# Four input loads moved to the head of the DMA queue, and two state updates moved ahead of a row split, at the start of the dense layer of a delta-rule and mixture-of-experts kernel

## The reference, cut to what matters

```
y[:, :, t] = einsum('bhd,bhde->bhe', q[:, :, t], state)
v_old = einsum('bhde,bhd->bhe', state, kt)
state = state + bt * einsum('bhd,bhe->bhde', kt, vt - v_old)
```

## Time and profile before

| | |
|---|---|
| median of 3 runs | 976.65 us (973.17, 976.65, 976.8) |
| the profiled execution | 976.8 us, span in the profile 975.1 us |
| PE busy | 922.7 us, 95% of the span |
| DVE, ACT, POOL busy | 459.7, 422.8, 193.9 us |
| DMA | 167.66 MB, mean 172 GB/s |

### The profile page before, as it was taken

The page is one execution under the profiler, slowest core; times in us unless marked ns, Lnnn a source line. Parts: engine busy times, 40 slices in busy tenths (PEclk is TensorE's granted clock), DMA queues, the critical chain, the costliest instruction groups (busy, mean ns, idle before and its releaser), DMA issues.

```text
span 975.1 us, 27207 instructions
## 1 busy us (share of the span) xinstructions
PE 922.7 (95%) x10970; PEld 787.3 (81%) x10971; DVE 459.7 (47%) x948; ACT 422.8 (43%) x765; POOL 193.9 (20%) x146
## 2 busy tenths in 40 slices
PE   4688999999999999999999999976999999999998
PEld 4687778888888788878888888764889899889997
DVE  6999579545855486457522252340232323222221
ACT  4126754654465346544643565511333333333332
POOL 3000000000000000000000052437266633376311
PEclk7689999999999999999999999977899999999999
DMA  7009748543753366435542868137356733362100
GB/s 318 4 27 355 280 164 292 236 131 132 249 214 131 123 223 235 143 120 186 184 153 99 277 226 299 48 138 229 135 205 232 266 129 137 129 260 74 64 22 8
DMA packets 33153, 167.66 MB, mean 172 GB/s; under 512 B 4862, under 2 KB 8100, under 8 KB 27170
## 3 DMA queue, kind: packets, MB, share of 16 engines
q1 hardware_dynamic: 26402, 136.47, 38.9%
q0 software_dynamic: 6560, 29.70, 8.4%
q10 hardware_dynamic: 96, 0.10, 0.0%
HBM read 143.04 MB, written 23.40 MB: 171 GB/s over the span
## 4 chain that ended last, share of the span: by engine, by line
PE 85%; DVE 7%; issue 3%; DMA 2%; ACT 1%; POOL 1%; ACTq 0%; DVEq 0%; POOLq 0%
PE HP L1232 7%; PE ACC L1245 7%; PE HP L1234 6%; PE HP L1233 6%; PE ACC L1246 6%; PE ACC L1247 6%; PE ACC L1651 5%; PE ACC L1650 5%; PE HP L1619 4%; PE ACC L1652 4%; PE HP L1620 4%; PE HP L1621 4%; PE P L1630 3%; PE P L1111 2%; PE P L1138 2%
## 5 line engine op out<-in xcount | busy, mean ns | idle before, releaser
L380 POOL TENSOR_TENSOR we_l<-raw_e,we_h 128x768 fp32r<-128x768 f32 x16 | 29.7, 1870 | 588.7 <-ACT we_h L516 588.7
L482 ACT ACTIVATE relu<-HP 128x512 f32<-128x512 f32 x96 | 57.4, 598 | 203.3 <-PE HP L1234 203.3
L798 DVE TENSOR_TENSOR h_l<-h,h_h 128x512 fp32r<-128x512 f32 x96 | 66.4, 692 | 158.3 <-ACT h_h L490 158.3
L1232 PE MATMUL HP<-x_h,ring 128*128 128x512 f32 x288 | 118.4, 411 | 1.6 <-DVE x_l L791 1.6
L1245 PE MATMUL ACC<-h_h,ring 128*128 128x512 f32 x288 | 116.9, 406 | 2.8 <-DVE h_l L798 2.8
L1233 PE MATMUL HP<-x_h,ring 128*128 128x512 f32 x288 | 113.2, 393 | 0.0
L1234 PE MATMUL HP<-x_l,ring 128*128 128x512 f32 x288 | 113.2, 393 | 0.0
L1246 PE MATMUL ACC<-h_h,ring 128*128 128x512 f32 x288 | 112.5, 391 | 0.0
L1247 PE MATMUL ACC<-h_l,ring 128*128 128x512 f32 x288 | 112.5, 391 | 0.0
L1650 PE MATMUL ACC<-we_h,hT_h 128*128 x240 | 84.7, 353 | 3.6 <-issue 3.4
L1461 POOL TENSOR_TENSOR we_l<-raw_e,we_h 128x1536 fp32r<-128x1536 f32 (+2 forms) x24 | 84.0, 3526 | 19.0 <-DMA we_h<-in_w 18.7
(11 more groups left out here) (222 smaller groups left out, 1723.7 us busy)
## 6 DMA issues: line engine op xcount, KB each, us to landing
ring<-w_scratch SPq DMA_DIRECT2D x80, 768.0 KB, 4.4
raw_e<-in_w SPq DMA_DIRECT2D x16, 1536.0 KB
w_scratch<-ring SPq DMA_DIRECT2D x16, 768.0 KB, 4.4
we_h<-in_w POOLq DMA_DIRECT2D x6, 1536.0 KB, 9.2
kT<-in_kT SPq DMA_DIRECT2D x6, 1024.0 KB, 8.1
kk<-in_k SPq DMA_DIRECT2D x6, 1024.0 KB, 6.7
qT<-in_qT SPq DMA_DIRECT2D x6, 1024.0 KB, 8.3
we_h<-in_w POOLq DMA_DIRECT2D x6, 1024.0 KB, 6.0
```

The costliest lines, as they stand in the source:

```text
L1232: pe.matmul(HP[n % 2][:, :], win_h[:, cols], x_h[:, k, :], start=k == 0, stop=False)
```

## The change

Two lists are reordered; no instruction is added, removed or changed in size.

On SP, the four input loads go ahead of all stores and loads of the weights. The first store and the first load of the loop are taken out of the small loop ahead of it, with the second pair now issued at `i = 0`.

On DVE, the two halves of `new_state(1, g)` are written ahead of `rows_lo(0)` instead of behind it.

```
@@ sync @@
         move_last_heads(sp, (0,))
-        for f in range(2):
-            store_pair(f)
-            load_pair(NPAIR + f)
+        keys_T(2)
+        values(1)
+        queries(1)
+        keys(2)
+        store_pair(0)
+        load_pair(NPAIR)
         for i in range(NF1 * NCH):
             dt, f = divmod(i, NF1)
             t = dt + 1
-            if 0 < i and i + 1 < NF1:
+            if i + 1 < NF1:
                 store_pair(i + 1)
                 if i + 1 + NPAIR < NF1:
                     load_pair(i + 1 + NPAIR)
-            if i == 0:
-                values(1)
-            elif i == 1:
-                keys(2)
-            elif i == 2:
-                keys_T(2)
-            elif i == 3:
-                queries(1)
@@ vector @@
         substitute(1, 9, 20)
-        rows_lo(0)
         for g in range(2):
             new_state(1, g)
+        rows_lo(0)
```

## The result

| | before | changed |
|---|---|---|
| median of 20 runs | 974.48 us (971.82 to 978.19) | 978.48 us (976.27 to 984.99) |
| ratio of the runs | | 1.0058, 95% interval 1.0045 to 1.0073 |
| the profiled execution | 976.8 us, span 975.1 | 982.32 us, span 980.6 |

The prediction was 977.5 and no measurable change, with 0.07 for slower. The median lies inside the range, but the ratio is clear of 1, and its middle is above the 1.005 that I had called the limit of what can be told (the interval reaches down to 1.0045). So the forecast was wrong in kind: the loss is about 5.6 us by the ratio, not 0.85. The same kernel run again in a later comparison gave 1.0038 (1.0022 to 1.0054), 3.7 us: smaller, but again clear of 1.

A forecast was written before the change was run, and what follows sets the result against it. PE, busy 95% of the span, was taken as the bound. Terms -0.1 (hidden inside the 0.65), +0.65 and +0.2 gave +0.85 us: 977.65 on the profiled 976.8, 977.5 against the median 976.65; range 973.0 to 980.1.

The forecast's parts named there:

- What bounds, and what there is to gain: Whole kernel: PE bounds, busy 95%; no engine waits for the four moved loads, so issuing them earlier gives nothing directly.
- (a) DVE's order: Around 73 us, state halves ahead of `rows_lo`: `up(0)` later, `h_l` 0.13 earlier; worth -0.1 us, bounds -0.33 and +0.3.
- the 0.65: Delay in us of `x_l` and `up(0)` from DVE's new order, claimed hidden by PE's following wait for `h_l`.
- (b) The landing of block 4: SP's queue: weight block 4, behind inputs and first store, lands at 86.0 us, bounds 84.5 and 88.5.
- the time until the engines are full: SP's queue: DMA engines full from 72.0 us, 0.9 us after the first issue at 71.14.
- the pace from there on: SP's queue once full: 0.365 MB/us, last engine's lag included, as at the kernel's start; 5.11 MB take until 86.0.
- the prediction's own rule: Block 4's landing delays ACT, then `h_l(2)` and `down(2)` beyond its slack: +0.65 us at 86.0, 3.1 at 88.5.
- What hangs on the landing: `relu(2)` 2.17 us late, `down(2)` +0.65, `below_blocks(1)` +0.2 more; the shift stays to the end.
- The clock: PE's granted clock: no fall in the forecast, longest idle 1.8 us; a fall costing 3.3 us only past about 88.
- the queue starves ACT, and PE's clock falls: Rival: queue at 0.295 MB/us, blocks 4 to 7 late, +4.5 us plus 3.3 from the clock, +7.8, 984.4; chance 0.07.
- The limit of what can be told: Whole kernel time: about 0.5%, 4.9 us, separates a measurable change from none; chance of the same 0.90.

The follow-up runs named there:

- Weights first: Changed kernel with the first store and the load of weight block 4 issued ahead of the four inputs; ratio 1.0011 to the kernel before.
- The dose kernels: Changed kernel with the load of `kk` behind block 4's load: 1.0006; changed kernel with block 1's store and block 5's load ahead of it: 1.0085.
- SP's order alone: Kernel before with only SP's reordering of loads and stores, DVE's list left in its old order; ratio 1.0054.

## Why the prediction was wrong

**What bounds, and what there is to gain.** Right. No wait was on the four inputs, and issuing them earlier gave nothing.

**(a) DVE's order.** Right as a mechanism: the wait moves from `down(0)` to `up(0)`. It moves by more than the 0.65: `up(0)` starts 2.5 us after the first `x_h` in the changed kernel and 1.5 before, since DVE ended `substitute` 0.75 us after that `x_h` began and not 0.34. -0.1 was forecast; the trace of this part alone has +0.5 in the stretch, the ratio 1.0014 does not differ from 1. I had not thought that the longer idle time ahead of `up(0)` could bring the clock down by itself; two of ten profiles have it.

**(b) The landing of block 4, where it failed.** The prediction lets block 4 land at 86.0, 14.9 us after the first issue at 71.14. It took 17.6, in the same terms 88.7, outside even the upper bound of 88.5. Two parts of that sum were wrong.

The first is the time until the engines are full, put at 0.9 us and so 1.3 below that of the start of the kernel. The changed kernel needed 2.7: its first load was issued at 70.33, and the windows have 154 and 221 GB/s before 426 from 73.0 on. That is +1.8 us. The 0.9 came from the window at 72 of the kernel before, whose queue begins with a store there. "Weights first", which begins with a store too, is full after 1.1 us; the profiles that begin with loads after 2.2 to 2.7, as at the start of the kernel. I had taken the figure of a queue in another order.

The second is the pace from there on. 5.11 MB took 14.9 us and not 14.0, +0.9. The row of loads at the start has no dip in it, and ours has three microseconds at 229, 229 and 301 GB/s ahead of the first store; against 415 that is 1.2 us by my estimate. Together the two parts are the 2.7 us that were missing. The other terms were right: the store at 2.15 us (2.3 without the lag), and the lag of the slowest engine, 1.5 us both in the start's 16.1 us (15 engines done with `vv` at 15.37, the last at 16.88) and here. The start's 16.1 us with nothing taken off would have given 87.3 and by the prediction's own rule some 2 us of loss.

**What hangs on the landing.** Right in kind and in each link: ACT, `relu(2)`, `h_l(2)`, `down(2)`, then the shift stays to the end. With the measured landing the rule of the prediction gives the loss without the clock: at 88.5 it said +3.1 for `down(2)`; 3.3 us of wait were measured, and 3.8 for the stretch with the clock held up. The dose kernels confirm it on both sides.

**The clock.** In the forecast it was absent, on the ground that at a landing of 86.0 PE's longest idle stretch would be 1.8 us; in the rival that I called "the queue starves ACT, and PE's clock falls" it was put at 3.3 us, from a landing "past about 88". This is what happened, in its first half: block 4 at 88.7, 3.3 us idle, 3.4 us of lost work behind it in the profile. The second half of the rival, a growing backlog with blocks 5 to 7 further behind, did not come; after the one dip the queue ran at over 400 GB/s, blocks 5 and 6 were 0.3 us late, and the total is +5.6 and not +7.8. So the rival deserved far more than 0.07. The fall of the clock that it cites from the earlier trace rows comes at 33.2 us in the trace, not at 33.6; nothing hangs on that. The clock doesn't fall behind this wait in every execution: of the two profiles of the changed kernel one has it; in the other it had fallen ahead of the wait, which was 1.3 us there. The runs reach from 976 to 985 us, with the lower granted clock in the longer ones, but where it fell in them is known only for the profiled ones. By the mean granted clocks, SP's order alone lost 2.4 us more work to the clock than the kernel before on the same chip, and the changed kernel run again 0.8, each to within about 1 us. The Trainium skill says on its page "TensorE: Matmul & The Clock Gate", in "Part 1: The HAM clock gate", that the moment of a transition varies from run to run since the monitor's cycle is not tied to the kernel's start. The traces agree: the fall came 2.5 us after PE had run out of work in the changed kernel, at 90.4, and 3.9 us after in SP's order alone, at 92.1, when PE was at work again; the waits were 3.3 and 3.6 us, and the lost work 3.4 and 1.7.

**The limit of what can be told.** 4.9 us was taken as the size that decides between the same and slower. With 3.8 from the wait and up to 2.9 from the clock in some runs, the effect, 5.6 us in one comparison and 3.7 in the other, lies right at this limit; a forecast of 3.8 alone would still have said the same.

## What to carry to other kernels

A load that nobody waits for is only free as long as what is queued behind it isn't needed either: price a reordered queue by the first critical transfer behind the moved ones, and compare the landing with the last moment at which it does no harm. Take the time until the engines are full from a queue that begins with the same kind of transfer, take the pace and the lag of the slowest engine from rows with both, and look for a dip where the first store follows loads. Where the answer lies within 2 us of that moment, bound it from the slow side, because a wait of PE is paid twice when the granted clock falls behind it. And an engine strictly in order, as ACT here, turns one late buffer into a delay of all the work behind it, so put the critical load first and the bulk after: the same traffic in the other order cost nothing measurable.

## What was not expected of the hardware

- Where the first store follows a row of loads, the queue fell to 229 to 301 GB/s for three microseconds with the DMA engines at full share, against some 400 to 460 for loads. The time was lost by the load ahead of the store (`kk`: 4.0 us and not 2.5), and the store itself ran at full pace. Two stores in a row had one such dip, and the store behind the next load, in the same backlog, none.
- A queue that began with 1 MB loads was full 2.2 to 2.7 us after its first issue (eight profiles, and the start of the kernel), one that began with a store of 768 KB after 1.1 us ("weights first").
- One of the 16 DMA engines was 1.2 to 1.8 us behind the other 15 in the landings that followed a 16 KB packet of the instruction queue (eight profiles). A load has landed only when the last engine is done, so block 4 took 17.6 us where 15 engines were done after 16.1.
- 16 unused matmuls in an idle gap kept the clock at 2.4 GHz there and came with a loss of 6.3 and 6.6 us at another place 340 us later, in the same place in both profiles: 2.9 and 3.2 us of idle PE without a releaser, and the clock behind it.
